# Three matmul layers behind attention, in fp32 by three passes: layer 1's squares on ScalarE, and another order of VectorE's additions in the second stages

## The reference

```python
# q, k, v: (2, 12, 448, 64);  w_in: (768, 2048), w_out: (2048, 768), for each of two MLPs
scores = cap * np.tanh(q @ k.T / 8 / cap)          # per batch and head
attn   = softmax(scores) @ v
x = attn.transpose(0, 2, 1, 3).reshape(896, 768)
r = np.maximum(x @ moe_w_in, 0.0);  x = (r * r) @ moe_w_out         # "layer 1", layer == 0 in the code
h = x @ moe2_w_in;                  out = (h * sigmoid(h)) @ moe2_w_out   # layer == 1 in the code
```

## Time and profile before

| | |
|---|---|
| median of 3 runs | 536.1 us (535.16 to 537.03) |
| the profiled execution | 535.17 us, of which 533.4 us from its first to its last instruction |
| TensorE busy | 521.4 us |
| VectorE busy | 351.5 us |
| ScalarE busy | 260.2 us |
| granted TensorE clock | 0.999 of full speed |

### The profile page before, as it was taken

The page is one execution under the profiler, slowest core; times in us unless marked ns, Lnnn a source line. Parts: engine busy times, 40 slices in busy tenths (PEclk is TensorE's granted clock), DMA queues, the critical chain, the costliest instruction groups (busy, mean ns, idle before and its releaser), DMA issues.

```text
span 533.4 us, 7052 instructions
## 1 busy us (share of the span) xinstructions
PE 521.4 (98%) x2628; PEld 439.9 (82%) x2628; DVE 351.5 (66%) x604; ACT 260.2 (49%) x404; POOL 77.5 (15%) x52
## 2 busy tenths in 40 slices
PE   7999999999999999999998999999999999999996
PEld 5333335799999999999998999999999999999896
DVE  3388888797777634667898746556764255568885
ACT  4999996154554333454443344545444145444220
POOL 1999999000000000000000000000000000000000
PEclk9999999999999999999999999999999999999999
DMA  8899611051202202412022024201210241021545
GB/s 220 197 236 233 173 40 35 26 143 55 80 0 80 59 1 63 136 59 80 0 80 60 1 60 138 60 28 52 67 57 15 60 138 57 6 78 37 104 69 79
DMA packets 82181, 42.17 MB, mean 79 GB/s; under 512 B 26848, under 2 KB 79072, under 8 KB 82144
## 3 DMA queue, kind: packets, MB, share of 16 engines
q1 hardware_dynamic: 77984, 40.32, 29.3%
q10 hardware_dynamic: 4128, 1.38, 1.1%
q0 software_dynamic: 32, 0.00, 0.0%
HBM read 38.93 MB, written 2.75 MB: 78 GB/s over the span
## 4 chain that ended last, share of the span: by engine, by line
PE 89%; DVE 4%; ACT 3%; issue 1%; DMA 1%; ACTq 0%; DVEq 0%
PE banks L558 26%; PE banks L557 26%; PE banks L559 26%; PE banks L477 4%; PE banks L470 4%; PE banks L498 2%; ACT prob L683 1%; PE banks L467 1%; ACT prob L690 1%; DVE w_hl L980 1%; DMA qk_raw<-in_q_dram 1%; PE banks L489 1%; DVE y L1060 1%; ACT prob L680 0%; DVE w_raw L994 0%
## 5 line engine op out<-in xcount | busy, mean ns | idle before, releaser
L557 PE MATMUL banks<-x_hi,w_hl 128*128 128x448 f32 x384 | 139.4, 363 | 0.0
L558 PE MATMUL banks<-x_lo,w_hl 128*128 128x448 f32 x384 | 139.4, 363 | 0.0
L559 PE MATMUL banks<-x_hi,w_hl 128*128 128x448 f32 x384 | 138.3, 360 | 0.0
L557 PE MATMUL banks<-g_hi,w_hl 128*128 128x448 f32 (+1 forms) x340 | 122.7, 361 | 2.7 <-DVE y L1060 2.7
L558 PE MATMUL banks<-g_lo,w_hl 128*128 128x448 f32 (+1 forms) x340 | 122.6, 361 | 0.0
L559 PE MATMUL banks<-g_hi,w_hl 128*128 128x448 f32 (+1 forms) x340 | 121.8, 358 | 0.0
L557 PEld LDWEIGHTS banks<-x_hi,w_hl 128*128 128x128 f32 x384 | 72.1, 188 | 6.9 <-issue 1.4
L559 PEld LDWEIGHTS banks<-x_hi,w_hl 128*128 128x128 f32 x384 | 71.8, 187 | 5.1
L558 PEld LDWEIGHTS banks<-x_lo,w_hl 128*128 128x128 f32 x384 | 72.1, 188 | 3.8
L557 PEld LDWEIGHTS banks<-g_hi,w_hl 128*128 128x128 f32 x340 | 63.8, 188 | 7.9 <-issue 3.4
L975 DVE TENSOR_TENSOR w_hl<-w_raw,w_hl 128x768 fp32r<-128x768 f32 x32 | 31.9, 998 | 55.4 <-ACT w_hl L716 55.2
(11 more groups left out here) (63 smaller groups left out, 509.6 us busy)
## 6 DMA issues: line engine op xcount, KB each, us to landing
w_raw<-in_moe_w_in_dram SPq DMA_DIRECT2D x32, 384.0 KB, 3.3
w_raw<-in_moe_w_out_dram SPq DMA_DIRECT2D x24, 512.0 KB, 5.3
qk_raw<-in_k_dram SPq DMA_DIRECT2D x44, 112.0 KB, 3.0
qk_raw<-in_q_dram SPq DMA_DIRECT2D x44, 112.0 KB, 3.5
v_t<-in_v_dram SPq DMA_DIRECT2D x24, 96.0 KB, 2.8
out_dram<-rows SPq DMA_DIRECT2D x38, 56.0 KB, 2.2
qk_raw<-in_k_dram ACTq DMA_DIRECT2D x4, 112.0 KB, 3.2
qk_raw<-in_q_dram ACTq DMA_DIRECT2D x4, 112.0 KB, 4.4
```

Source lines behind the costliest of these rows:

```text
L557: pe.matmul(dst, hi[:, kk, :], mov_hi, start=start, stop=False, skip_group_check=onto)
L558: pe.matmul(dst, hi[:, kk, :], mov_lo, start=False, stop=False, skip_group_check=onto)
L559: return pe.matmul(dst, lo[:, kk, :], mov_hi, start=False, stop=stop, skip_group_check=onto)
```

## The change

In `layer == 0` the squares are ScalarE activations (Square, in place) directly behind the two Relus, and VectorE's `relu_squared` is gone. In the second stages VectorE's order is another: `take(g,0)` and, in group 1, the additions of group 0 stand ahead of `w_s4` and of the `leave` calls, and all `leave` calls of group `g` - 1 go further back. With `s` = 0 the two orders are the same, since there `leave` does nothing and these `take` calls are absent. TensorE's, SyncE's and GpSimd's programs are not touched.

```diff
@@ ScalarE, hidden_act @@
                     act.activation(work[2 * (p % 2) + b][:, :], ring[2 * (p % 2) + b][:, 0:S],
                                    ACT.Relu if layer == 0 else ACT.Silu).then_inc(s_h[layer], 1)
+                if layer == 0:
+                    for b in range(B):
+                        act.wait_ge(s_h[0], B * (SF * s + p) + b + 1)
+                        w = work[2 * (p % 2) + b]
+                        act.activation(w[:, :], w[:, :], ACT.Square).then_inc(s_square, 1)
@@ VectorE @@
-            def relu_squared(s, p):
-
-                for b in range(B):
-                    dve.wait_ge(s_h[0], B * (SF * s + p) + b + 1)
-                    w = work[2 * (p % 2) + b]
-                    dve.tensor_tensor(w[:, :], w[:, :], w[:, :], ALU.mult).then_inc(s_square, 1)
-
...
-                            if layer == 0:
-                                relu_squared(s, p - 1)
...
-                    if layer == 0:
-                        relu_squared(s, SF - 1)
...
                     prod_low(layer, s, 1, 1)
-                    leave(layer, s, 0, 0)
-                    leave(layer, s, 0, 1)
                     take(layer, s, 0, 5)
                     if s == 1:
                         prod_low(layer, s, 1, 2)
...
                     for g in range(1, GROUPS):
                         last = g == GROUPS - 1
                         end = last and layer == 1 and s == 1
+                        if s == 0 or g > 1:
+                            prod_low(layer, s, g, 2)
                         if s == 1:
                             take(layer, s, g - 1, 6)
-                        if s == 0 or g > 1:
-                            prod_low(layer, s, g, 2)
+                            take(layer, s, g, 0)
                         w_s4(layer, s, g)
-                        leave(layer, s, g - 1, 2)
-                        if s == 1:
-                            take(layer, s, g, 0)
                         prod_low(layer, s, g, 3)
-                        leave(layer, s, g - 1, 3)
+                        if g == 1:
+                            leave(layer, s, 0, 0)
+                            leave(layer, s, 0, 1)
                         if s == 1:
                             take(layer, s, g, 1)
                         prod_low(layer, s, g, 4)
+                        leave(layer, s, g - 1, 2)
                         if s == 1:
                             take(layer, s, g, 2)
                         prod_low(layer, s, g, 5)
+                        leave(layer, s, g - 1, 3)
```

## The result

The changed kernel takes 533.03 us (median of 5 runs, 532.54 to 533.39), the kernel before 535.16 (5 runs, two more than the prediction had, whose median was 536.1): a ratio of 0.9956 with a 95% interval of 0.9944 to 0.9967, so 2.4 us faster with 1.8 to 3.0 (the two medians themselves are 2.1 us apart). The profiled span went from 533.4 to 530.7 us, which is the -2.7 of the sum; how far that is luck is said behind the experiments.

The account below looks back on a forecast made before the run. The prediction took TensorE's program and its two pauses at product (1, 2) to bound the kernel. -3.15 (moved additions) + 0.45 (squares) = -2.70 us, from a median of 536.1 to 533.4 us, range 532.3 to 535.1.

Parts of the forecast that it names:

- the sum: The predicted change of the whole kernel: -3.15 + 0.45 = -2.70 us.
- What bounds the kernel: TensorE's program and pauses alone count; two pauses at product (1, 2), one per s = 1 stage, 1.59 + 1.56 us.
- The moved additions, -3.15: In the second stages with s = 1, additions onto y come earlier on VectorE and both TensorE pauses go: -3.15 us.
- The margin at product (1, 2), 0.70: After the move, the addition that product (1, 2) waits for is seen by TensorE 0.70 us before it is due.
- The squares, +0.45 at tile 2: At the first stage's start, two squares push tile 2's weights by 0.92 us: a new TensorE pause, +0.45 us.
- 1.36 to spare against 0.92: In layer 0's second stages, t_sum's g_low has 1.36 us to spare against the squares' push of 0.92: no cost.
- The later stores, put at nothing: SyncE's stores of groups 0 and 1 go out up to 5 us later, before the last group's; no term.
- 2.0 us to spare: In the steady course of tiles, two links of ScalarE and VectorE take 12.4 us of 14.4, so nothing is late.
- rival 4: Table switches forth and back at every tile, 2.57 us per hidden_act, 19 + 2.6 us of cost: 555 us; chance 0.04.
- 1: Rival: one table load of 1.28 us before the first squares, where tile 2 waits: 534.7 us; chance 0.08.
- 2: Rival: a pause at product (1, 2) closes only in part or in one stage, -1.1 us: 535.0 us; chance 0.07.
- 3: Rival: the pauses at product (1, 2) stay, released by something that moves with take(1,0): +0.45, 536.6 us; chance 0.05.

Follow-up runs that it names:

- squares_only: The kernel before with only the squares moved to ScalarE, VectorE's order of the second stages as before; 535.78 us, ratio to before 1.0011.
- leaves_back: The changed kernel with leave(0,0) and leave(0,1) back ahead of take(0,5), in both layers; ratio to before 0.9968.
- first_squares_back: The changed kernel, but for tile 0 of the first stage ScalarE copies tile 2's weights first and squares behind that; 532.44 us, ratio to before 0.9951.
- dose1: first_squares_back with one unread copy on ScalarE behind the squares of every first-layer tile but tile 0; +0.89 us over it between first and last matmul.
- switch: The changed kernel with Exp and Silu in place of each tile's two squares; 464.28 us from first to last matmul, 35.1 more than the changed kernel.
- leaves_early_in_last: first_squares_back with group 1's leave calls early again in group 2 of the stages with s = 1; 532.35 us, ratio to before 0.9941.
- moves_only: The changed kernel with the squares back on VectorE, so the moved additions alone; 532.74 us, ratio to before 0.9955.
- dose4: first_squares_back with four unread copies on ScalarE behind the squares of every first-layer tile but tile 0; 447.69 us from first to last matmul, 19.0 more.

## Why the prediction came out right, and what in it did not hold

- **What bounds the kernel: right.** 18.2 us off VectorE gave nothing (`squares_only` is slower than before); only the two pauses counted.
- **The moved additions, -3.15: right,** -3.16 measured alone. The margin at product (1, 2), 0.70, was 0.69, and `leaves_back` tested it from the other side: its pauses were 0.37 and 0.35, against 0.38.
- **The squares, +0.45 at tile 2: right in place and cause, 0.05 too much.** A pair of squares costs 0.93 us from start to start (0.92 forecast). What was mis-sized is the signal: `tile_low(2)` ended at 106.98 + 0.96 = 107.94 and its matmul started at 107.99, 0.05 later, and the next one 0.11 late. I had 0.15 and then 0.08 more.
- **No cost of the squares in the second stages, "1.36 to spare against 0.92": right.** `first_squares_back`, with the squares there, has no pause. But this was the wrong instruction to look at: the weights of product (0, 2) are ready only 0.70 us ahead, less than the 1.36, and `take(0,2)` 0.38 ahead of product (0, 4).
- **The later stores, put at nothing: wrong.** The prediction let them go out "all of them before the last group's" and gave them no term. They hold SyncE's queue, and its last store starts 0.5 us later: 4.77 against 4.44 us from the last matmul to the end, +0.3 in the sum.
- **"2.0 us to spare" in the steady course: wrong,** without effect on the time. The spare time is 1.21 us for a pair, since both tiles of a pair are in one loop. The step that failed is the one that set the odd tile's Relus 0.2 us behind its end whatever happened before. By it, rival 4 would decide at 1.0 us per `hidden_act`; by the loop it does at about 0.6 for the tiles, and `dose1`, with 0.46, was already late in the second stages. Its price was too low for the same reason: 19 + 2.6 us forecast, 35.1 measured for the loads of `switch`.
- **Rivals.** No table load was added (the two of before, at the first Exp, L665, and at L748, are all there are), so 1 and 4 did not occur. The Trainium skill ("ScalarE: Activation LUTs", Table sets: the hidden batching unit) doesn't name square among the functions that are in every set; the trace here shows that it is in the one that Exp, Tanh, Relu and Copy were using:

```profile
L754 ACT ACTIVATE work<-work 128x448 f32<-128x448 f32 x32 | 16.7, 580 | 0.0
```

2 and 3 did not occur either: no wait for an addition is left.
- **The rule of the Trainium skill** ("ScalarE: Activation LUTs", Rules for kernel authors), multiplications to VectorE, is given there with VectorE's speed in bf16. Here, in float32, a square takes 0.58 us on ScalarE and 0.62 on VectorE, so that reason has no hold, but the rule's outcome has, by another way. As far as the time goes this half of the change is a loss of 0.4 us, cured by one copy's place or by leaving the squares where they were.
- **From 2.7 to the measured 2.4.** The difference lies within the interval, but the traces have a cause of its size. Between the matmuls the change is -2.75, and the later end gives 0.33 back: -2.4. That the profiled span shows -2.7 is luck: its stages began 0.28 us earlier, and nothing in the change touches attention. The ratios of the runs fit this: for `leaves_early_in_last`, without the late stores, 0.9941 is 3.2 us, as between the matmuls, while those of the four kernels with them stand for 0.2 to 0.8 us less than between the matmuls; each of these ratios alone is unsure by some 0.6 us. The forecast of 533.4 itself stood on a median of 536.1, 0.9 above that of five runs.

The best version tried is `leaves_early_in_last`, 532.35 us: no pause of TensorE is left in its stages, and its end is as early as before. `moves_only` and `first_squares_back` have no pause either, but the later end.

## What to carry to other kernels

When one engine is busy without a break, read the distances between its starts, not the busy times: each pause belongs to one place in another engine's queue, and its gain ends with the pause, however much is moved. Work moved to a half-idle engine is free or not by where it stands in that engine's queue, and the margin has to be worked out around the whole loop (who releases the next round?), not along one link. A dose of dummy work at single places measures such margins, one run for each place. And the end of a kernel has a queue of its own: what is put off to shorten a wait can fill it.

## What the runs showed of the hardware that was not expected

TensorE's clock fell in the two kernels with long pauses. Windows of `dose4` with the columns of the earlier trace rows, behind the pause that ended at 141.26:

```profile
139.00:141.20 2.20, 0.14 (x1) 0.00 (x0) 0.96 (x2) 1.67 (x4) 0.00 (x0) 1.00 0.00 0
141.20:144.40 3.20, 3.14 (x8) 2.81 (x9) 1.70 (x3) 2.63 (x6) 0.00 (x0) 0.50 0.00 0
```

A granted clock of 0.50 is the 1.2 GHz level, and a matmul came every 0.37 us there instead of every 0.20. It was back after about 3.2 us, so that the matmuls took some 1.5 us more. The pause of equal length that ended at 258.45 had no such fall behind it (clock 1.00 in 256.00 to 260.00). In `switch` it fell behind the four pauses of 3.5 to 4.0 us (clock 0.50 in 128.66 to 134.05, in 165.75 to 171.50 and in 253.69 to 256.70, and 0.53 in 291.00 to 294.60) and not behind one of 2.7 (1.00 in 271.90 to 275.00) or one of 2.4 (1.00 in 299.20 to 303.00). All pauses under 2 us, in all kernels, were followed by matmuls 0.20 us apart. Why one pause of 2.3 us differs from another was not tried.

In `dose4` the lost 1.5 us came back whole. Tile 6 and product (0, 0) behind it, in the first stages with the fall and without:

```profile
141.26 0.74 PE L560 MATMUL banks<-x_hi,w_hl 128*128 128x448 f32 x1 [2.11 <-DVE w_hl L995]
157.56 0.47 PE L560 MATMUL banks<-g_hi,w_hl 128*128 128x448 f32 x1
...
258.45 0.47 PE L560 MATMUL banks<-x_hi,w_hl 128*128 128x448 f32 x1 [2.11 <-DVE w_hl L995]
274.75 0.47 PE L560 MATMUL banks<-g_hi,w_hl 128*128 128x448 f32 x1 [1.62 <-DVE w_hl L1000]
```

It is 16.30 us from one to the other both times. The slow matmuls only filled what would have been the next pause, since the loop over ScalarE and VectorE was what set the pace. In `switch` it is the same: 18.78 and 18.79 us from tile 4 to tile 6, though the clock was down for 5.4 us in one and 3.0 in the other.
